# Second unit's dots, turning and mask moved in front of and inside the first head of a clustered-attention kernel

## The reference

```python
q_assign = np.argmax(np.einsum('bhsd,hcd->bhsc', q_n, c_n), axis=-1)
k_assign = np.argmax(np.einsum('bhsd,hcd->bhsc', k_n, c_n), axis=-1)
mask = q_assign[:, :, :, None] == k_assign[:, :, None, :]
scores = scale * np.matmul(q, k.transpose(0, 1, 3, 2))
scores = np.where(mask, scores, -1000000000.0)
attn = np.exp(scores - np.max(scores, axis=-1, keepdims=True))
attn = attn / (np.sum(attn, axis=-1, keepdims=True) + 1e-09)
return np.matmul(attn, v).astype(np.float32)
```

## Time and profile before

| | us |
|---|---|
| median of 3 timed runs | 688.76 |
| lowest, highest | 687.22, 689.47 |
| profiled execution, its own time | 687.45 |
| its span, first to last instruction | 685.6 |
| PE busy in the span | 674.9 |
| DVE, ACT, POOL busy | 341.6, 276.2, 232.7 |
| mean granted clock of PE | 0.995 |

### The profile page before, as it was taken

How to read it: one execution, slowest core, us unless ns; L and a number is a source line. 1 busy time by engine, 2 the same in 40 slices (tenths; PEclk the granted TensorE clock), 3 DMA queues, 4 the chain that set the end, 5 groups by cost and what they waited for, 6 DMA issues and landing times.

```text
span 685.6 us, 9772 instructions
## 1 busy us (share of the span) xinstructions
PE 674.9 (98%) x3666; PEld 549.2 (80%) x3666; DVE 341.6 (50%) x662; ACT 276.2 (40%) x586; POOL 232.7 (34%) x253
## 2 busy tenths in 40 slices
PE   7899999999999999999999999999999999999998
PEld 6677776767676789888888888888888899988886
DVE  4887786877876649633113111141111489944300
ACT  5767676767767613111111111121111387734411
POOL 5745878658595050887200000000150070000000
PEclk8999999999999999999999999999999999999999
DMA  5563544425444101344000000010230620000111
GB/s 172 146 151 83 137 141 108 118 65 149 118 128 111 58 1 32 96 119 108 16 1 1 0 1 0 1 62 0 76 109 1 185 62 0 1 32 15 47 47 46
DMA packets 26494, 47.04 MB, mean 69 GB/s; under 512 B 3792, under 2 KB 10832, under 8 KB 26448
## 3 DMA queue, kind: packets, MB, share of 16 engines
q1 hardware_dynamic: 23392, 38.08, 19.9%
q0 software_dynamic: 2912, 7.95, 3.7%
q10 hardware_dynamic: 144, 0.39, 0.2%
HBM read 35.98 MB, written 3.15 MB: 57 GB/s over the span
## 4 chain that ended last, share of the span: by engine, by line
PE 95%; DVE 4%; ACT 0%; issue 0%; POOL 0%; DVEq 0%; POOLq 0%
PE ps L1616 19%; PE ps L1582 19%; PE ps L1664 10%; PE ps L1678 10%; PE ps L1375 10%; PE ps L1361 9%; PE ps L1345 6%; PE ps L1346 5%; PE ps L1462 2%; PE ps L1297 1%; PE ps L1390 1%; PE ps L1517 1%; PE ps L1432 1%; PE ps L1601 1%; PE ps L1314 1%
## 5 line engine op out<-in xcount | busy, mean ns | idle before, releaser
L1175 DVE SCALAR_TENSOR_TENSOR hid_l<-ps,hid_h 128x512 fp32r<-128x512 f32 x48 | 33.2, 691 | 196.6 <-ACT hid_h L819 196.6
L819 ACT ACTIVATE hid_h<-ps 128x512 fp32r<-128x512 f32 x48 | 28.7, 598 | 223.7 <-PE ps L1582 223.7
L1361 PE MATMUL ps<-cst,prob 128*128 128x128 f32 x576 | 81.3, 274 | 0.9 <-DVE pt L945 0.9
L1345 PE MATMUL ps<-k,q 80*128 80x384 f32 x192 | 75.5, 393 | 1.1 <-ACT prob L706 0.8
L1616 PE MATMUL ps<-w_h,hid_h 128*128 128x512 f32 x192 | 76.2, 397 | 0.0
L1616 PE MATMUL ps<-w_h,hid_l 128*128 128x512 f32 x192 | 75.5, 393 | 0.0
L1616 PE MATMUL ps<-w_l,hid_h 128*128 128x512 f32 x192 | 74.7, 389 | 0.0
L1361 PEld LDWEIGHTS ps<-cst,prob 128*128 128x128 f32 x576 | 67.4, 141 | 8.8 <-issue 1.8
L1375 PE MATMUL ps<-pt,v_n 128*64 128x384 f32 x384 | 68.8, 494 | 0.0
L1346 PE MATMUL ps<-k,q 128*128 128x384 f32 x192 | 66.1, 344 | 0.0
L937 DVE TENSOR_REDUCE row_min<-ps 128x1 f32<-128x768 f32 x64 | 61.0, 954 | 7.8 <-PE ps L1346 6.8
(11 more groups left out here) (181 smaller groups left out, 1451.0 us busy)
## 6 DMA issues: line engine op xcount, KB each, us to landing
w_raw<-in_moe_w_ch SPq DMA_DIRECT2D x24, 256.0 KB, 2.6
raw_d<-in_q SPq DMA_DIRECT2D x8, 384.0 KB, 3.4
v_n<-in_v SPq DMA_DIRECT2D x16, 192.0 KB, 2.5
out<-out_s SPq DMA_DIRECT2D x12, 256.0 KB, 2.0
raw_qk<-in_k SPq DMA_DIRECT2D x15, 192.0 KB, 3.2
raw_qk<-in_q SPq DMA_DIRECT2D x15, 192.0 KB, 3.6
q<-q SPq DMA_DIRECT2D x15, 192.0 KB, 3.2
k<-k SPq DMA_DIRECT2D x15, 192.0 KB, 3.7
```

Of the source, the lines that this page charges most:

```text
L1345: nc.tensor.matmul(bank, q2[s][0:D + C, cols], k2[s][0:D + C, keys], start=True, stop=False)
L1361: last = nc.tensor.transpose(ps[:, 4 + hf, j * P:(j + 1) * P], prob[t % 2][:, R * hf + j, :], ident)
```

## The change

Only the first 30 us of the program are written differently.

- SP loads the raw queries and keys of unit 1 into buffers of their own (`raw_e`), ahead of v of head 0, k and q of head 1. Its later load of the same data (`load_dots(1)`) goes.
- For unit 0, DVE finds the hits in two halves as before, but weighs, takes the largest weight and makes the masks on whole rows.
- PE: nine idle matmuls in place of four ahead of `turn_mask(0)`, then `dots(1)` at once, two idle matmuls in place of three, and `turn_dots(1)` between the scores of tiles 0 and 1. `turn_mask(1)` comes one step earlier. The dots of unit 1 use PSUM bank 6 instead of 7.
- ACT stores unit 1's dots ahead of `store_mask(0)` and of the first exponent.
- DVE takes unit 1's largest dots, hits and first hits ahead of step 0, its masks ahead of step 1.

POOL's stream is unchanged.

```diff
+        raw_e = [sb(pre, f"raw_e{j}", [S]) for j in range(2)]
...
             sp.wait_ge(raw_d_loaded[1], 16)
+            for j, t in enumerate((q_t, k_t)):
+                sp.dma_start(raw_e[j][:, :], pair_of(t, 1)).then_inc(raw_e_loaded[j], 16)
             load_v(0, 0)
...
             sp.wait_ge(k_split, 1)
-            load_dots(1)
             sp.dma_start(stage[:, 0, 0], w1[0, :, :]).then_inc(w1_raw_loaded[0], 16)
...
             place_q_rows(0)
+            store_dots(1)
             store_mask(0)
             exponent(0, 0, 0)
-            store_dots(1)
...
-            first_masks(0)
-            first_masks(1)
+            first_hits(0)
+            first_hits(1)
+            dve.wait_ge(half_hit, 1)
+            weigh_hits(0)
+            first_hit(0)
+            masks(0)
...
             place_k_rows(0)
-            for t in range(2):
-                minimum(0, 0, t)
+            minimum(0, 0, 0)
+            largest_dot(1)
+            minimum(0, 0, 1)
+            hits(1)
+            first_hit(1)
             step(0, 0, 0)
-            largest_dot(1)
-            hits(1)
+            masks(1)
             step(0, 0, 1)
-            first_hit(1)
-            masks(1)
             step(0, 0, 2)
...
-            keep_busy(4)
+            keep_busy(9)
             turn_mask(0)
-            keep_busy(3)
+            dots(1)
+            keep_busy(2)
             scores(0, 0, 0)
+            turn_dots(1)
             scores(0, 0, 1)
-            dots(1)
             step(0, 0, 0)
-            turn_dots(1)
             step(0, 0, 1)
+            turn_mask(1)
             step(0, 0, 2)
-            turn_mask(1)
             step(0, 0, 3)
```

More of the change, by code:

```diff
@@ L208, in build @@
         half_dots, half_max, half_hit = sem("half_dots"), sem("half_max"), sem("half_hit")
-        half_weighed, half_first = sem("half_weighed"), sem("half_first")
         q2_first, k1_first, k2_first = sem("q2_first"), sem("k1_first"), sem("k2_first")
@@ L223, in build @@
         raw_d_loaded = [sem(f"raw_d_loaded{j}") for j in range(2)]
+        raw_e_loaded = [sem(f"raw_e_loaded{j}") for j in range(2)]
         q2_masked = [sem(f"q2_masked{s}") for s in range(2)]
@@ L344, in dots_bank, with unit_dots @@
             return 4 if u == 0 and j else 7
+        def unit_dots(u):
+            return ps[:, 6 if u == 1 else 7, 0:4 * NT * C]
         def mask_place(t, tp):
@@ L686, in store_dots @@
                 act.wait_ge(hit_max_done, u)
-                nc.scalar.activation(hit_w[:, :, :].rearrange("p n c -> p (n c)"), ps[:, 7, 0:HALF],
+                nc.scalar.activation(hit_w[:, :, :].rearrange("p n c -> p (n c)"), unit_dots(u),
                                      ACT.Copy).then_inc(dots_stored, 1)
@@ L946, in store_right, with first_hits @@
                                       ps[:, 5, 0:HALF].rearrange("p (j c) -> p j c", j=R)).then_inc(right_stored, 1)
-            def first_masks(j):
+            def first_hits(j):
                 part = slice(2 * NT * j, 2 * NT * (j + 1))
@@ L958, in first_masks, with dots_v @@
                                         ALU.is_equal).then_inc((half_hit, hit_done)[j], 1)
[L959 to L972, removed]
+            def dots_v(u):
+                return unit_dots(u).rearrange("p (n c) -> p n c", c=C)
             def largest_dot(u):
                 dve.wait_ge(dots_turned, u)
-                nc.vector.tensor_reduce(dot_max[:, :], dots_v, axis=AX.X, op=ALU.max).then_inc(dot_max_done, 1)
+                nc.vector.tensor_reduce(dot_max[:, :], dots_v(u), axis=AX.X, op=ALU.max).then_inc(dot_max_done, 1)
             def hits(u):
                 dve.wait_ge(dot_max_done, u + 1)
-                nc.vector.tensor_tensor(hit[:, :, :], dots_v,
+                nc.vector.tensor_tensor(hit[:, :, :], dots_v(u),
                                         dot_max[:, :].unsqueeze(2).broadcast_to([P, 4 * NT, C]),
@@ L999, in masks @@
                 for j, op in enumerate((ALU.is_equal, ALU.not_equal)):
-                    top = hit_max[:, :].rearrange("p (a j m) -> p a j m", a=R, j=2)[:, :, j, :]
+                    if u:
+                        top = hit_max[:, :].rearrange("p (a j m) -> p a j m", a=R, j=2)[:, :, j, :]
+                    else:
+                        top = hit_max[:, :].rearrange("p (j a m) -> p j a m", a=R, j=2)[:, j, :, :]
                     nc.vector.tensor_tensor(
@@ L1288, in dots @@
             def dots(u):
-                pe.wait_ge(mask_stored, u)
-                pe.wait_ge(hit_done, u)
+                if u > 1:
+                    pe.wait_ge(mask_stored, u)
+                    pe.wait_ge(hit_done, u)
                 for j in range(2):
-                    pe.wait_ge(raw_d_loaded[j], 16 * (u + 1))
-                    tiles = raw_d[j][:, :].rearrange("p (a b c) -> p a b c", a=R, b=2)
+                    if u == 1:
+                        pe.wait_ge(raw_e_loaded[j], 16)
+                    else:
+                        pe.wait_ge(raw_d_loaded[j], 16 * u)
+                    tiles = (raw_e if u == 1 else raw_d)[j][:, :].rearrange("p (a b c) -> p a b c", a=R, b=2)
                     for tp in range(2):
                         at = 2 * C * (2 * j + tp)
-                        last = nc.tensor.matmul(ps[at:at + 2 * C, 7, 0:HALF], cen_b[:, u // 2, :], tiles[:, :, tp, :],
+                        last = nc.tensor.matmul(unit_dots(u)[at:at + 2 * C, :], cen_b[:, u // 2, :], tiles[:, :, tp, :],
                                                 start=True, stop=True)
@@ L1305, in turn_dots @@
                 for a in range(R):
-                    last = nc.tensor.transpose(ps[:, 7, a * P:(a + 1) * P], by_group[:, a * P:(a + 1) * P], ident)
+                    last = nc.tensor.transpose(unit_dots(u)[:, a * P:(a + 1) * P], by_group[:, a * P:(a + 1) * P],
+                                               ident)
                 last.then_inc(dots_turned, 1)
@@ L1312, in turn_mask @@
                 pe.wait_ge(mask_ready, 2 * u + 2)
+                if u == 1:
+                    pe.wait_ge(mask_stored, 1)
                 for a in range(R):
```

## The result

| | before | changed |
|---|---|---|
| median of 20 runs, us | 688.80 | 690.76 |
| lowest, highest | 687.01, 691.33 | 688.91, 692.00 |
| profiled execution, its own time | 687.45 | 690.42 |
| its span | 685.6 | 688.6 |
| DVE's first reduction of head 1 | 27.78 | 30.89 |

The ratio of the changed kernel to the one before is 1.0025 (95% interval 1.0014 to 1.0036): slower by 0.25%, which is 1.7 us, clear of zero and within the 0.3% that the prediction took as its bound. The two profiled executions differ by 3.0 us.

A forecast was written before the change was run, and what follows sets the result against it. Head 0 was taken as bound by DVE, the rest by PE. The wait for POOL (+0.7) and one cold PE step (+1.1) gave +1.8 us: 689.25 from the profiled execution, 690.6 from the median, middle 689.9, range 687.4 to 692.0.

The forecast's parts named there:

- The wait for POOL: DVE's first hit of unit 1 waits 1.5 to 3.5 us for POOL's weighing; PE waits 2.5 to 4 us.
- When POOL is free: Early loads delay head 1's q by +0.8 us (bounds 0 to 2.0); POOL's split ends 19.4, first hit starts 20.45.
- DVE from there: DVE's pieces from first hit to head 1's first reduction sum to 8.00 us; head 1 starts at 28.45, +0.7 us.
- The half clock behind the rest: PE rests 2.6 to 3.9 us, its clock falls between 21 and 22.5; one cold step costs +1.1 us.
- rival C: Clearly slower: q 1.5 to 2 us late, first hit at 21.5, half clock 6.8 us; +4.2, 692; chance 0.20.
- Sum: Whole change: 0.7 + 1.1 = +1.8 us; 689.25 from the profiled execution, 690.6 from the median, middle 689.9.
- the signs to look for: Profile after: among others, POOL's weighing starts at 18.6 to 20 and head 1's first reduction at 28 to 30 us.
- Unit 0 on whole rows: DVE's fewer, longer instructions for unit 0 leave the first mask at the same time, 0.1 us either way.
- Nine idle matmuls: Ahead of the first mask's turning on PE: take 2.57 us, end at about 10.86, clock stays full through tiles 0 and 1.
- The early half clock as a consequence of PE's rest: Before, the clock halved between 10.5 and 11 us after PE rested from 9.43; staying full speeds eight score matmuls by 1.4 us.
- What the rest of the change is worth: Without the wait for POOL, the warm start and shorter DVE stretch would gain 1.6 to 2.6 us.
- rival B: Faster: POOL's weighing ends by about 18.7, so the gain stays; -1.6 to -2.6 us, 686.5; chance 0.10.

The follow-up runs named there:

- a5: Changed kernel, but DVE weighs unit 1's hits itself with weights from PSUM and POOL's weighing goes; 687.70 us, ratio 0.9990 to the kernel before.
- c4: Changed kernel with POOL's weighing of unit 1's hits moved ahead of its two operations on head 1's keys; 687.57 us, ratio 0.9983 to the kernel before.
- a4: Changed kernel with unit 1's first hits and masks back behind DVE's step 1, their turning behind PE's step 2; 687.04 us, ratio 0.9978.
- a2: Changed kernel with unit 1's raw queries and keys loaded behind v, k, taps and q of head 1; 689.34 us, ratio 1.0012 to the kernel before.
- c2: Kernel before with only the early loads of unit 1's raw queries and keys added; 688.86 us, ratio 0.9997 to the kernel before.
- a3: Changed kernel with PE's rest ahead of turning tile 1's right half filled by 11 idle matmuls; 689.94 us, ratio 1.0025 to the kernel before.
- b3: Kernel before with nine idle matmuls instead of four ahead of the first mask's turning; 688.14 us, ratio 0.9999 to the kernel before.
- a6: The version of a4 with four idle matmuls instead of nine ahead of the first mask's turning; 689.22 us, ratio 1.0002 to the kernel before.
- a1: Changed kernel, but DVE weighs unit 1's hits itself with weights from SBUF and POOL's weighing goes; 689.06 us, ratio 1.0004 to the kernel before.

## Why the prediction was right, and where it was off

**The wait for POOL: right.** It named the place (first hit, behind POOL's split of head 1), what is queued behind it, and PE's wait. Measured 3.18 us on DVE and 3.30 on PE. The minimum of tile 2, whose scores were there at 18.6, started at 22.12, right behind first hit. With this the trace agrees with the rule of the Trainium skill (TensorE: Matmul & The Clock Gate, "Architectural detail: the array is 16× 32×32, not 1× 128×128") that DVE's queue is strictly first in, first out. a5, c4 and a4 take the wait away or shorten it in three manners, and each returns 3.1 to 3.7 us by the medians, 2.4 to 3.2 by the ratios; so the cause, this wait with the half clock behind it, is shown.

**When POOL is free: right in kind, mis-sized.** The term "I take +0.8 us" measured +1.97, the upper bound. The estimate had the pair landing at 10.4 and each later transfer 0.6 to 1.2 us behind. The pair landed at 10.7 and v at 11.6, as estimated; but k came at 12.6 and q at 14.0, 1.0 and 1.4 us behind the one ahead. So first hit started at 21.65, not 20.45. That the early pair is what delays q is shown both ways: with the loads behind q (a2) POOL started at 11.99, with them early in the kernel before (c2) at 13.76. The large transfers landed in the order of issue. This fits the rule of the Trainium skill (DMA: Bandwidth & Descriptors, "Two DMAs through the same engine are not ordered") that descriptors of one queue start in order on an engine.

**DVE from there: right.** 8.00 us of pieces were predicted from first hit to head 1; 9.24 - 1.18 of idle time = 8.06 were measured, and 7.98 in a2, a3, a5 and c4.

**The half clock behind the rest: right, its size in part by luck.** +1.1 us was taken, 1.18 measured as DVE's waits, and a3 removes them. The clock fell at 22.6 and lasted to 29.5. But the price was reckoned as "one step", and nearly all of two steps of PE (24.8 to 29.8) ran at half clock. Both waits stand in the first of them; ahead of the second DVE had the key rows of unit 1 to place (1.15 us), and it did not wait. By the words of rival C ("as soon as two or more steps of PE run at half clock") this would have been the clearly slower case.

**Rival C: its condition came, its time did not.** It had q 1.5 to 2 us late and first hit at 21.5; measured were 1.97 and 21.65. Of its 1.7 + 2.5 the first term is about what the trace shows (1.9), the second was 1.2.

**Sum.** 0.7 + 1.1 = 1.8 was predicted for the shift of head 1, 3.1 measured; 1.2 of the missing 1.3 is the transfer of q. The forecast of 689.9 came within 0.9 us of the median, 690.76, partly by luck: half of the 1.31 us by which the profiled execution lay below the median had been added, and these 0.65 made up for half of what was missing. Two of the signs to look for were missed with the same term: POOL's weighing started at 20.62 (18.6 to 20 expected), head 1 at 30.89 (28 to 30).

**Unit 0 on whole rows, "0.1 us either way": wrong.** b3 and a5 have the same timing here, their second halves begin at 9.38, and the masks are done at 11.30 in halves and at 12.04 on whole rows: +0.74. The first half's weighing, largest weight and mask had used the time in which the second half's dots were awaited; on whole rows they come behind it.

**Nine idle matmuls, "end at about 10.86": wrong in this execution.** They took 3.79 us at half clock, not 2.57, and ended after the masks (12.04), which were turned only at 12.79. The prediction had the clock at full from 8 to 18 us. Neither slip shows in the result, since the wait for POOL lies behind both.

**The early half clock as a consequence of PE's rest: wrong.** The prediction read the fall at 10.75 us as brought about by the rest from 9.43. In the changed kernel the granted clock fell at 9.0, in c4 at 9.9 and in b3 at 7.7, and in all three PE had worked without a rest since the dots began (at 6.37, 6.47 and 5.74). Nine idle matmuls did not hold it. What they go with is an earlier return: to full at 12.4 in the changed kernel and 14.5 in b3, against 17.6 in the kernel before and 16.6 in a6 with four. So the scores of tiles 0 and 1 did run at full clock, as forecast.

**What the rest of the change is worth: less than rival B had.** In a5, c4 and a4, where POOL's wait is gone or short, the kernel is 0.7, 1.2 and 1.5 us faster than before by the ratios, against the 1.6 to 2.6 of rival B. The interval of a5 includes no gain. Which part brings it, the early dots or the earlier full clock, is not separated.

## What to carry to other kernels

When a step is moved forward on one engine, look where its producer stands in the other engine's queue: here POOL's weighing stood behind five operations that waited for a transfer, and the change also put 768 KB ahead of that transfer. If an instruction may have to wait, leave behind it only what needs it: with the first hit two steps later (a4) and nearly all else alike, the kernel is 3.7 us faster by the medians. Fill an engine's wait with a fixed number of idle instructions only after working out their time at either clock.

## What the runs showed of the hardware

- DVE's weighing with two SBUF inputs, begun beside a POOL operation that reads SBUF, took 2.07 us and ended 0.41 after POOL's end; with one input in PSUM it took 0.56 (a1, a5). Two SBUF inputs alone do not cost that: in the trace of a1 DVE's product of the gate (line 1242, 128x768, both inputs in SBUF) takes 0.95 us with POOL idle (at 601.07) and 2.05 beside POOL (at 561.93). The Trainium skill (SBUF — State Buffer, "SBUF: two separate sides") states this: the port pair that the two engines share is taken for a whole instruction, and the other one blocks. The trace agrees in both places.
- PE's pace at the start of an execution differs from one execution to the next. In the profile of a4 the nine idle matmuls took 4.19 us, the mask was turned at 15.60, and its execution took 690.10 where the median of a4 is 687.04. PE's timeline of a4:

```profile
6.47 5.33 PE L1287 MATMUL ps<-cen_b,raw_d 128*128 128x32 f32 x24 [0.57 <-DVE cen_b L925]
11.62 4.19 PE L1442 MATMUL ps<-cen_b 128*128 128x128 f32 x18
15.60 0.85 PE L1324 MATMUL ps<-cst,mask_n 128*128 128x128 f32 x3
```

  The same 24 dot matmuls took 2.98 us in the changed kernel.

- The granted clock in a profile can read 1.00 while PE works at half pace. The nine idle matmuls of b3 took the same 4.19 us; there the stretch reads 0.50, in a4 it reads 1.00. PE's timeline of b3, then a stretch of b3 and the same of a4:

```profile
9.16 4.19 PE L1432 MATMUL ps<-cen_b 128*128 128x128 f32 x18
```
```profile
12.00:13.00 1.00, 1.00 (x7) 1.00 (x6) 0.00 (x0) 0.00 (x0) 0.83 (x1) 0.50 0.73 276
```
```profile
12.00:13.00 1.00, 1.00 (x6) 1.00 (x6) 0.86 (x3) 0.00 (x0) 0.00 (x0) 1.00 0.90 232
```

  At the start, then, the durations are the measure, not the column.

- The mean granted clock of each execution tells the two sorts apart, with few exceptions. Of the 99 executions of the kernel before that were timed beside the experiments, the 23 with 1.000 took 689.8 to 691.2 us (median 690.5); the median of the other 76 is 688.4. Of the changed kernel's twenty, four have 1.000 (median 691.2), and the median of the others is 690.6. Like with like, and across different rounds, the change costs about 2.2 us in one sort and 0.7 in the other. The executions of one kernel spread over 2 to 5 us; effects of 1 us are read from the trace's pieces, not from two total times.
